# Attention, routed experts and a feed-forward layer in one kernel: first block begun on two turns' scatters, ten tiles of tokens put in another order

## The reference

```
attention   k, v averaged over groups of 8 positions (72 keys); softmax(q k / 8) v
experts     x = attention output, (2304, 512)
            noisy = x @ w_gate + log1p(exp(x @ w_noise)) * noise      # 8 experts
            top 2 of 8, weights = softmax over the two
            out[token] = sum over its two experts  w_k * relu(x @ w1[e]) @ w2[e]    # 512 -> 1024 -> 512
last layer  h = x @ w_in; g = max(0.01 h, h); out = g @ w_out                       # 512 -> 2048 -> 512
```

## Time and profile before

| what | value |
|---|---|
| median of 3 runs | 1105.24 us |
| time of the profiled execution | 1103.91 us |
| its span | 1102.2 us |
| mean granted TensorE clock | 0.967 |
| busy TensorE / VectorE / ScalarE / GpSimd | 94% / 34% / 25% / 34% |
| attention, to the last product of a tile (L561) | 0 to 113.3 us |
| first product of block 0 (L603) | 141.55 us |
| last product of the last block | ends about 677.3 us |
| first product of the last layer | 692.71 us |

### The profile page before, as it was taken

How to read it: one execution, slowest core, us unless ns; L and a number is a source line. 1 busy time by engine, 2 the same in 40 slices (tenths; PEclk the granted TensorE clock), 3 DMA queues, 4 the chain that set the end, 5 groups by cost and what they waited for, 6 DMA issues and landing times.

```text
span 1102.2 us, 16369 instructions
## 1 busy us (share of the span) xinstructions
PE 1033.5 (94%) x5180; PEld 870.6 (79%) x5181; DVE 378.9 (34%) x678; ACT 272.5 (25%) x497; POOL 379.6 (34%) x413
## 2 busy tenths in 40 slices
PE   5988289999999999999999995899999999999998
PEld 4887268888888888888888884788888888888887
DVE  5988542122212221222122212653333333333222
ACT  3443012222222222222222220232222222222222
POOL 3338691280917355371908202950100100000000
PEclk9988589999999999999999997899999999999999
DMA  8945452151524333251514212421101101001000
GB/s 296 337 145 189 178 160 77 57 180 39 171 67 140 97 111 127 80 158 49 173 63 144 95 38 72 147 78 39 39 20 58 39 20 58 20 1 39 1 1 38
DMA packets 53779, 105.75 MB, mean 96 GB/s; under 512 B 7408, under 2 KB 7536, under 8 KB 53744
## 3 DMA queue, kind: packets, MB, share of 16 engines
q1 hardware_dynamic: 35312, 63.33, 18.1%
q10 hardware_dynamic: 12672, 23.07, 6.3%
q0 software_dynamic: 5760, 18.88, 5.1%
HBM read 77.47 MB, written 27.79 MB: 95 GB/s over the span
## 4 chain that ended last, share of the span: by engine, by line
PE 79%; issue 9%; DVE 7%; POOL 3%; DMA 1%; ACT 1%; SPq 0%; POOLq 0%; DVEq 0%; ACTq 0%
PE ps L603 23%; PE ps L605 23%; PE ps L604 23%; PE ps L629 3%; POOL w_split L467 2%; PE ps L561 2%; PE ps L610 1%; PE ps L539 1%; POOL w_split L465 1%; PE ps L671 1%; DVE maxima L906 1%; PE ps L549 1%; DVE x L1149 1%; DVE k_sum L892 1%; DMA k_raw<-in_kT_dram 1%
## 5 line engine op out<-in xcount | busy, mean ns | idle before, releaser
L467 POOL TENSOR_TENSOR w_split<-w_raw,w_split 128x512 fp32r<-128x512 f32 x144 | 186.3, 1294 | 12.0
L465 POOL TENSOR_SCALAR w_split<-w_raw 128x512 fp32r<-128x512 f32 x144 | 92.3, 641 | 226.7 <-PE ps L605 224.7
L603 PE MATMUL ps<-w_split,xs_hi 128*128 (+1 forms) x344 | 138.4, 402 | 3.9 <-DVE xs_lo L1108 3.9
L603 PE MATMUL ps<-w_split,hT_hi 128*128 (+1 forms) x344 | 139.0, 404 | 2.0 <-DVE hT_lo L1115 2.0
L605 PE MATMUL ps<-w_split,hT_lo 128*128 (+1 forms) x344 | 135.4, 394 | 0.0
L605 PE MATMUL ps<-w_split,xs_lo 128*128 (+1 forms) x344 | 134.7, 391 | 0.0
L604 PE MATMUL ps<-w_split,hT_hi 128*128 (+1 forms) x344 | 134.6, 391 | 0.0
L604 PE MATMUL ps<-w_split,xs_hi 128*128 (+1 forms) x344 | 134.6, 391 | 0.0
L492 POOL DMA_INDIRECT y_in<-y_blocks,y_rows x36 | 34.8, 968 | 269.1 <-DVE x L1149 194.8
L603 PE MATMUL ps<-x_hi,w_split 128*128 128x512 f32 (+1 forms) x320 | 120.5, 377 | 1.4 <-DVE x_lo L1157 1.4
L604 PE MATMUL ps<-x_lo,w_split 128*128 128x512 f32 (+1 forms) x320 | 118.8, 371 | 0.0
(11 more groups left out here) (147 smaller groups left out, 1505.3 us busy)
## 6 DMA issues: line engine op xcount, KB each, us to landing
w_raw<-in_wall_dram SPq DMA_DIRECT2D x160, 256.0 KB
xs<-x_sorted ACTq DMA_DIRECT2D x45, 256.0 KB, 2.7
y_blocks<-y_sb ACTq DMA_DIRECT2D x43, 256.0 KB, 2.0
k_raw<-in_kT_dram SPq DMA_DIRECT2D x16, 288.0 KB, 5.5
q_sb<-in_qT_dram SPq DMA_DIRECT2D x18, 256.0 KB, 5.2
v_raw<-in_vT_dram SPq DMA_DIRECT2D x16, 288.0 KB, 5.2
out_dram<-h_sb SPq DMA_DIRECT2D x10, 256.0 KB, 2.0
x_sorted<-zero_rows SPq DMA_DIRECT2D x9, 256.0 KB, 4.1
```

Of the source, the lines that this page charges most:

```text
L465: pool.tensor_scalar(hi, w_raw[:, a, :], 1.0, 0.0, ALU.mult, ALU.add).then_inc(split_hi, 1)
L467: pool.tensor_tensor(lo, w_raw[:, a, :], hi.bitcast(F32), ALU.subtract).then_inc(split, 1)
L603: pe.matmul(out_ap, lhs_hi, rhs_hi, start=first, stop=False)
```

## The change

- SyncE's queue: all 16 chunks of stage 0 and the nine zero stores stand ahead of the load of q 15. GpSimd splits all 16 chunks before the first scatter.
- The scatters of turns 0 and 1 (22) count on `x_sent_early`, the other 14 on `x_sent_late`; SyncE turns the two into `x_landed` 1 and 2. Block 0's load waits for `first_needs`, which is 1 if expert 0 has at least 128 rows after two turns, and 2 otherwise.
- TensorE makes up(0), turn_h(0), down(0) with nothing between; turn_rows(1) is in the middle of down(0), and block 1's load waits for all scatters. VectorE does split_rows(0) ahead of the lists and list_y_rows behind split_h(1).
- Ten tiles of tokens (1280) get a new order: tokens that need none of the last eight blocks come first. `find_early` on VectorE flags them and adds them up by tile, two products on TensorE (`rank_tokens`) rank them, `place_tokens` gives each its place. A record of 32 bytes a token (two rows of y, two weights, the token's number) is stored to that place by ten indirect DMAs and read back in one.
- Tiles 0 and 1 of the new order are gathered when 35 blocks are stored, before stage 8's splits; they are mixed in the last but one block and turned before the last down. Stage 9's splits start when the last block is done, and tile 2's gather follows its second chunk. PSUM banks move for this.
- The outputs of groups 0 to 2 are stored by indirect DMAs on GpSimd, by the token numbers.

The orders at both ends of the block loops are written out:

```diff
+EARLY_TURNS = 2
+EARLY_SENT = 2 * TURN_FROM[EARLY_TURNS]
+RECORD = 8
+UNROLLED = 2
+SCAN = 16
+MOVED_GROUPS = 3
+MOVED = OUT_FROM[MOVED_GROUPS]
+LAST_BLOCKS = MOVED - OUTS[0]
+LATE_ROW = (BLOCKS - LAST_BLOCKS) * P
...
-        y_rows = sb("y_rows", [P, TILES, 2], I32)
-        mix = sb("mix", [P, TILES, 2])
+        record = sb("record", [P, TILES, RECORD], I32)
+        mix = record[:, :, 2:4].bitcast(F32)
...
+
+        def x2_bank(tile):
+            return (7, 4)[tile] if tile < OUTS[0] else 6 + tile % 2
...
-            sp.wait_ge(zeros_made, 1)
-            for row in ZEROED:
-                sp.dma_start(x_sorted[row:row + P, :], zero_rows[:, :]).then_inc(x_zeroed, 16)
...
             load_w(8)
+            load_v(13)
+            load_w(9)
             load_q(13)
-            load_v(13)
+            load_w(10)
             load_v(14)
-            load_w(9)
+            load_w(11)
+            sp.wait_ge(zeros_made, 1)
+            for row in ZEROED[0:4]:
+                sp.dma_start(x_sorted[row:row + P, :], zero_rows[:, :]).then_inc(x_zeroed, 16)
             load_q(14)
+            load_w(12)
             load_v(15)
-            load_w(10)
+            load_w(13)
+            for row in ZEROED[4:]:
+                sp.dma_start(x_sorted[row:row + P, :], zero_rows[:, :]).then_inc(x_zeroed, 16)
+            load_w(14)
+            load_w(15)
             load_q(15)
-            load_w(11)
             load_q(16)
             load_q(17)
-            for n in range(12, CHUNKS):
+            for n in range(CHUNKS, CHUNKS + RING):
                 load_w(n)
-            with sp.Fori(1, STAGES) as s:
+            sp.wait_ge(x_sent_early, 16 * EARLY_SENT)
+            sp.sem_inc(x_landed, 1)
+            sp.wait_ge(x_sent_late, 16 * (2 * TILES - EARLY_SENT))
+            sp.sem_inc(x_landed, 1)
+            for n in range(CHUNKS + RING, 2 * CHUNKS):
+                load_w(n)
+            for n in range(2 * CHUNKS, 3 * CHUNKS):
+                load_w(n)
+            sp.wait_ge(records_sent, 16 * MOVED)
+            sp.dma_start(record[:, 0:MOVED, :], records.rearrange("(t p) c -> p t c", p=P)).then_inc(records_back, 16)
+            with sp.Fori(3, STAGES) as s:
...
+                        in_=x_rows[:, tile, :], in_offset=None).then_inc(
+                            x_sent_early if turn < EARLY_TURNS else x_sent_late, 16)
...
+            for n in range(CHUNKS):
                 split_chunk(n)
-            n = SPLIT_FIRST
             for turn in range(len(TURNS)):
-                rows = rows_of(turn)
-                for at in range(0, len(rows), 2):
-                    send_rows(turn, rows[at:at + 2])
-                    if n < CHUNKS:
-                        split_chunk(n)
-                        n += 1
+                send_rows(turn, rows_of(turn))
...
+            await_last_use(2)
+            for c in range(CHUNKS):
+                split_next(2, c, 0)
+            pool.wait_ge(tokens_numbered, 2)
+            pool.wait_ge(records_made, 1)
+            for tile in range(MOVED):
+                pool.indirect_dma_start(
+                    out=records[:, :], out_offset=bass.IndirectOffsetOnAxis(ap=slots_i[:, tile, 0:1], axis=0),
+                    in_=record[:, tile, :], in_offset=None).then_inc(records_sent, 16)
+            await_last_use(3)
+            for c in range(CHUNKS):
+                split_next(3, c, 2 * STAGE)
+            with pool.Fori(2, EXPERTS // 2) as j:
...
+
+            def gather(t, y_from):
...
+            def send_out(g):
+
+                for m in range(OUTS[g]):
+                    pool.wait_ge(o_copied_dve if m % 2 else o_copied_act, OUT_FROM[g] // 2 + m // 2 + 1)
+                    pool.indirect_dma_start(
+                        out=out[:, :], out_offset=bass.IndirectOffsetOnAxis(ap=record[:, OUT_FROM[g] + m, 4:5], axis=0),
+                        in_=o_sb[m], in_offset=None).then_inc(o_placed[m], 16)
+
+            pool.wait_ge(records_back, 16)
+            pool.wait_ge(y_out, 16 * (BLOCKS - LAST_BLOCKS))
             for t in range(OUTS[0]):
-                gather(t)
+                gather(t, y_blocks[0:LATE_ROW, :])
+            await_last_use(EXPERTS)
+            for c in range(CHUNKS):
+                split_next(EXPERTS, c, 0)
             done = OUTS[0]
+            pool.wait_ge(blocks_done, BLOCKS)
             for c in range(CHUNKS):
                 split_next(EXPERTS + 1, c, 2 * STAGE)
                 if c + 1 in MIX_AT:
-                    gather(done)
+                    if done == OUTS[0]:
+                        pool.wait_ge(y_out, 16 * BLOCKS)
+                    gather(done, y_blocks[:, :])
                     done += 1
+            for g in range(MOVED_GROUPS):
+                ahead = OUT_FROM[g + 2] + 2
+                for t in range(done, ahead):
+                    gather(t, y_blocks[:, :])
+                done = ahead
+                send_out(g)
...
+                    if first and k == KF // 2:
+                        turn_rows(b + 1)
...
+            def rank_tokens():
+                pe.wait_ge(early_known, 1)
+                pe.matmul(token_ranks, before[:, :], is_early[:, :], start=True, stop=False)
+                pe.matmul(token_ranks, ones[:, :], tiles_ahead[:, :], start=False, stop=True).then_inc(tokens_ranked, 1)
...
+                if step == 1:
+                    pe.wait_ge(y_copied, BLOCKS)
...
+            turn_rows(0)
+            up(0, 0)
+            turn_h(0)
+            down(0, 0, True)
+            pe.wait_ge(lists_ready, 1)
+            up(1, expert_of(1))
+            turn_rows(2)
+            turn_h(1)
+            up(2, expert_of(2))
+            turn_rows(3)
+            rank_tokens()
+            down(1, expert_of(1), False)
+            turn_h(2)
+            with pe.Fori(3, BLOCKS - UNROLLED) as b:
+                up(b, expert_of(b))
+                turn_rows(b + 1)
+                down(b - 1, expert_of(b - 1), False)
+                turn_h(b)
+            for b in range(BLOCKS - UNROLLED, BLOCKS):
+                up(b, expert_of(b))
+                turn_rows(b + 1)
+                down(b - 1, expert_of(b - 1), False)
+                turn_h(b)
             for t in range(OUTS[0]):
                 turn_x2(t)
+            down(BLOCKS - 1, EXPERTS - 1, False)
+
...
-            act.wait_ge(x_sent, 16 * 2 * TILES)
+            act.wait_ge(first_known, 1)
+            needed = act.value_load(first_needs[0:1, 0:1], min_val=1, max_val=2)
+            act.wait_ge(x_landed, needed)
             act.dma_start(xs[:, :], x_sorted[0:P, :]).then_inc(xs_in, 16)
+            copy_rows(0)
+            relu(0)
+            copy_h(0)
             act.wait_ge(lists_ready, 1)
-            copy_rows(0)
+            act.wait_ge(x_landed, 2)
             load_rows(1)
...
+            for b in range(BLOCKS - UNROLLED, BLOCKS):
+                relu(b)
+                copy_rows(b + 1)
+                load_rows(b + 2)
+                store_rows(b - 1)
+                copy_h(b)
             for j in range(OUTS[0]):
                 copy_x2(0, j)
+            store_rows(BLOCKS - 1)
+
...
+                    if PLACE_AT.index(step) == EARLY_TURNS - 1:
+                        dve.tensor_scalar(first_needs[:, :], row_of[0:1, 0:1], float(P), 1.0, ALU.is_lt,
+                                          ALU.add).then_inc(first_known, 1)
...
+            split_rows(0)
...
+                then(dve.tensor_copy(record[:, :, 0:2], slots_f[:, :, :]))
...
+            def find_early():
+
+                then(dve.tensor_reduce(last_y[:, :], slots_f[:, 0:MOVED, :], axis=AX.X, op=ALU.max))
+                then(dve.memset(early_to[:, :, 0:SCAN], 0.0))
+                then(dve.tensor_scalar(is_early[:, :], last_y[:, :], float(LATE_ROW), None, ALU.is_lt))
+                then(dve.tensor_copy(early_to[:, 0, SCAN:], is_early[:, :]))
+                for n, back in enumerate((1, 2, 4, 8)):
+                    then(dve.tensor_tensor(early_to[:, 1 - n % 2, SCAN:], early_to[:, n % 2, SCAN:],
+                                           early_to[:, n % 2, SCAN - back:SCAN - back + MOVED], ALU.add))
+                dve.tensor_tensor(tiles_ahead[:, :], early_to[:, 0, SCAN:], is_early[:, :],
+                                  ALU.subtract).then_inc(early_known, 1)
+
+            def place_tokens():
+
+                dve.wait_ge(tokens_numbered, 2)
+                then(dve.scalar_tensor_tensor(out=place_late[:, :], in0=is_early[:, :], scalar=-1.0, in1=from_last[:, :],
+                                              op0=ALU.add, op1=ALU.mult))
+                dve.wait_ge(tokens_ranked, 1)
+                then(dve.tensor_tensor(place_f[:, :], token_ranks, place_late[:, :], ALU.subtract))
+                dve.wait_ge(x_sent_early, 16 * EARLY_SENT)
+                dve.wait_ge(x_sent_late, 16 * (2 * TILES - EARLY_SENT))
+                dve.tensor_copy(slots_i[:, 0:MOVED, 0], place_f[:, :]).then_inc(records_made, 1)
...
```

(36 more changed lines are left out.)

162 lines of the change are left out of this document (77 added, 85 removed).

## The result

The changed kernel has a median of 1110.57 us over 5 runs (1109.96 to 1110.96), the one before 1103.90 us over 5 (1102.44 to 1105.32): a ratio of 1.0061, 95% interval 1.0047 to 1.0075. It is 6.7 us slower; the forecast was 13 us faster. The profiled execution took 1110.74 us, its span 1109.0.

What follows compares the result with a forecast made beforehand. TensorE, busy 94% of the 1102.2 us span, bounds the kernel; only its waits and low-clock time can be won. 1103.9 - 1.0 (first joint) - 12.8 (second joint) = 1090.1, with 1.3 for the median 1091.4, said as 1091; range 1082 to 1100.

Steps and rivals of the forecast that it cites:

- First joint: Start of block 0, before the first transpose of sorted rows: earlier start, less a new wait and clock losses, +1.0 us.
- A second term: Attention stage: later q 14 and q 15 loads and moved zero stores count as nothing, 1 us either way each.
- The wait at the token ranks: First joint, TensorE at rank_tokens waiting for VectorE's early_known: 10 us of the gain turn into this new wait.
- Second joint: From T, the end of the last down, into the first group's products: early gathers of tiles 0 and 1 win 12.8 us.
- the third turn: Second joint, turn_x2(2): its gather is issued only behind chunk 1, a new wait of 3.4 us.
- In the middle: Blocks between the joints: unchanged 12.26 us each, with the ten record stores and place_tokens hidden.
- The +1 for the two turns ahead of the last down: Second joint: two transposes fill most of the pause before the last down, which had lost nearly 2 us; +1 us.
- rival (b): GpSimd paces all of group 0; with 5 us there and find_early at 6.8 us, 1099 us; chance 0.14.
- (c): Scatters come too late, after a late last split, delaying load 1: first joint -17.3 us, time 1109.7 us; chance 0.06.
- (a): VectorE's chain at the first joint is short: first joint +7 us, time 1085 us; chance 0.14.
- (d): Early gathers are not early because something on GpSimd stands before them; only the first joint is left, 1104 us; chance 0.05.
- the signs that the prediction names for being wrong: First block starts after 130, no wait shows at the ranks, or GpSimd's last-stage splits end later than T+50.

Runs made afterwards that it cites:

- run 78: Not a run label: in the quoted forecast, turn 0's 12 scatters "run 78 to 93" us instead of 70 to 97.
- The breaks: Changed kernel with a 2 us GpSimd memset behind each pair of scatters of turns 0 and 1: 1101.03 us, 9.5 us less than the changed kernel.
- experiment 4: Changed kernel with the earlier kernel's attention-stage order (8 chunks split first, the rest between scatter pairs, SyncE's queue as before): 1092.69 us, ratio 0.9897.
- experiment 5: Edits on experiment 4's kernel: ranks one block later 1082.72 us; last down ahead of two turns 1092.83; records spread 1092.16; ranks and records 1081.41, without early start 1101.55.
- experiment 6: Kernel before plus 16 scatters behind stage 1's splits: unbroken 1105.17 us (rerun 1113.64), in pairs 1104.08, as plain DMAs 1104.31; changed kernel with unbroken scatters and other additions 1118.79.

## Why the prediction was wrong

**The step that failed** is in "First joint": "Turn 0's 12 scatters then run 78 to 93 instead of 70 to 97; turn 1's slots come at 97.8 either way", and "Turns 2 and 3 start with their slots as before, so 'all landed' stays at 136.0". The scatters did run 76.2 to 91.4, and the 16th chunk was split by 76.0 against 78. But the slots come at the end of a chain in which TensorE, ScalarE and VectorE hand each other a tile's work, and hand-overs from TensorE beside a long row came 1.5 to 6 us late. I counted the row as busy time of GpSimd alone and gave it no other price; with before's order back, the rest of the change being the same, 17.9 us come back.

A second term failed with it: "the nine zero stores leave a stretch of busy queues for a less busy one. I count both as nothing; 1 us of gain or loss each in the range." Tile 10 is done 5.2 us late in the changed kernel, with no late increment before it. It is so in every trace: its rows of x are written at 80.6 to 82.3 in the nine with the new order, at 75.2 to 78.2 in the eleven with the old one. From 65 to 70 us the mean share of busy DMA engines is 1.00 against 0.50 before, and TensorE's granted clock 0.50 against 0.66; which of the moved loads, splits and zero stores does it is open.

In the changed kernel these two parts are 5.2 us up to tile 10 and 11.5 from there to the last tile, 16.7 of the 19.6 lost at turn_h(2). The breaks take away the second part, but only 9.5 us of time come back. The breaks make the last scatter late, and block 1's rows are loaded at 145.67 in place of 138.20 in experiment 4. TensorE's granted clock is a mean of 0.81 over the first 200 us against 0.87 before; what this costs is inside both parts and was not measured by itself.

Could it be read in the trace before? Its rows of 6 and 14 scatters lie where TensorE has few products to hand over, and there it shows no late start. Only their landings were a sign: of the 320 increments of the last 20 scatters the trace records 126, of the 256 of the first 16, which go in pairs, 207.

**What was right.** Block 0 starts from its own rows as soon as TensorE is free: 125.65 in experiment 4, forecast 125.8. The wait at the token ranks: 9.26, forecast about 10; with it gone 10.0 us are won. Second joint 13.6 us, forecast 12.8; the third turn waited 3.76 us against 3.4; the last hidden(0,3) ended at T+15.3 against T+13.1, with T at 695.7. In the middle 12.26 us a block; over all 40 of them the change loses 0.8 us, experiment 4 with the same record stores 0.2, and nothing is lost when they are spread.

**Mis-sized.** The first joint with before's order is -2.1 us (turn_h(2) ends 179.4 against 177.3), forecast +1.0: the late start at block 0's relu is in it. The +1 for the two turns ahead of the last down was no gain of its own (experiment 5).

**A misread line.** L1098 does not run "in a pause between splits", as the prediction has it for VectorE's neighbours. In the kernel before, beside it from 146.20, stands

```profile
146.20 0.83 POOL L465 TENSOR_SCALAR w_split<-w_raw 128x512 fp32r<-128x512 f32 x1
```

which took 0.62 us in each of the four chunks from 136.18 to 141.99. So here GpSimd's operation was the longer one and VectorE's was not. Only the 6.8 us in rival (b) lean on that reading.

**The rivals.** (c) gave 1109.7, close to the result, by another mechanism: scatters late because of late chunks. The chunks were early; it was right only in that the scatters would be late, and that its number is near is luck. It got a chance of 0.06. (a), (b) and (d) did not happen. Of the signs that the prediction names for being wrong, the first came true: block 0 starts at 142.49, after 130.

## What to carry to other kernels

Indirect DMAs in a row on GpSimd are not free for the others even where GpSimd has time: from some 4 us into the row TensorE's hand-overs came late in these runs, the last of them up to 3 us behind its end. Where a trace shows this, keep rows to a few, put GpSimd's other work (about 2 us for two to six scatters) between them; where a `remote` releaser shows up on a single core, look for such a row beside it. Work moved ahead of such a row is not free either: the new order had cost 5 us at tile 10, without a late increment. A new wait that the forecast itself names, like the one at the ranks, is the next thing to move: one block later, it gave 10.0 us.

## What the runs showed of the hardware

- Beside 16 indirect DMAs of 128 rows of 512 bytes in 20 us, TensorE's increments came up to 12.6 us late in one job and not at all in another, with the same program: 1113.64 against 1105.17 us. The two jobs were on two chips, and only one job ran on the chip without late increments; that it is the chip, and not something else of that job, is not shown. The experiments fell on five chips; four showed late increments, and the fifth ran only the first three kernels of experiment 6. The changed kernel was not run there, so its time on that chip is open.
- It is not the bytes alone: beside ten record stores without a pause, of 32 bytes a row, TensorE's increments came up to 3 us late (ScalarE waited 5.2 us in the changed kernel, 6.6 in experiment 4).
- Of VectorE's and ScalarE's own increments, none that the traces record beside these rows is over 0.25 us late. Whether plain DMAs from GpSimd hold anything is open: they were tried only on the chip that holds nothing. The mechanism itself is not shown, only its conditions. Every execution on record comes with a span and a granted clock, so none shows that TensorE's increments come late, or that the time is lost, when nothing is recorded.
